# Attention followed by two expert layers on one core: the drain of attention and the first two steps behind it in another order

## The reference, cut to what matters

```python
# attention: B, H, S, D = 2, 8, 768, 64; n_global = 8, n_local = 96
scores = q @ k.T / 8 - slope[h] * dist          # masked to a band of 96 keys and 8 global keys
a = softmax(scores)                             # exp(scores - max) / (sum + 1e-9)
x = (a @ v), heads side by side                 # 1536 x 512, float32
# two layers, each on 1536 tokens, d_model 512, d_ff 2048
h = x @ w_in;  g = h * sigmoid(h);              x = g @ w_out
h = x @ w_in2; g = h * clip(h + 3, 0, 6) / 6;   y = g @ w_out2
```

## Time and profile before

| | |
|---|---|
| median of 3 runs | 621.78 us (621.23 to 623.08) |
| the profiled execution, its own time | 621.76 us |
| its span in the trace | 619.6 us |
| PE busy | 595.8 us, 96% of the span |
| DVE, ACT, POOL busy | 370.6, 339.8, 283.6 us |
| mean granted TensorE clock | 0.989 of full speed |
| share of PE in the chain that ended last | 93% |

### The profile page before, as it was taken

How to read it: one execution, slowest core, us unless ns; L and a number is a source line. 1 busy time by engine, 2 the same in 40 slices (tenths; PEclk the granted TensorE clock), 3 DMA queues, 4 the chain that set the end, 5 groups by cost and what they waited for, 6 DMA issues and landing times.

```text
span 619.6 us, 9570 instructions
## 1 busy us (share of the span) xinstructions
PE 595.8 (96%) x3408; PEld 514.6 (83%) x3408; DVE 370.6 (60%) x696; ACT 339.8 (55%) x657; POOL 283.6 (46%) x353
## 2 busy tenths in 40 slices
PE   3999998599999999999999999999999999999998
PEld 2566666599999999899999998888888888888886
DVE  4778875645755576657655668557555685555431
ACT  3888884444444475544444756555556575555441
POOL 2888975723943333439533333377333333331110
PEclk9999999599999999999999999999999999999999
DMA  7444430212122212321322122212221242211002
GB/s 275 177 154 147 164 115 3 75 65 68 47 90 68 69 35 68 103 69 35 96 72 67 39 69 69 71 66 69 68 69 68 69 165 73 69 68 35 1 0 103
DMA packets 14883, 50.08 MB, mean 81 GB/s; under 512 B 1904, under 2 KB 2160, under 8 KB 14832
## 3 DMA queue, kind: packets, MB, share of 16 engines
q1 hardware_dynamic: 14832, 49.42, 23.4%
HBM read 46.27 MB, written 3.15 MB: 80 GB/s over the span
## 4 chain that ended last, share of the span: by engine, by line
PE 93%; DVE 3%; ACT 1%; issue 1%; DMA 1%; POOL 0%; DVEq 0%; SPq 0%; ACTq 0%
PE ps L898 37%; PE ps L977 22%; PE ps L968 14%; PE ps L969 7%; PE ps L870 4%; PE ps L845 4%; PE ps L855 4%; DMA words<-in_n_loc 1%; DVE x_lo L444 1%; DVE g_lo L586 1%; DVE wi_lo L435 0%; ACT probs L649 0%; POOL probs L274 0%; DVE g_f L460 0%; ACT g_hi L780 0%
## 5 line engine op out<-in xcount | busy, mean ns | idle before, releaser
L365 POOL TENSOR_TENSOR wo_lo<-wo_raw,wo_hi 128x1024 fp32r<-128x1024 f32 x32 | 76.6, 2393 | 282.4 <-ACT wo_hi L774 282.4
L898 PE MATMUL ps<-x_hi,wi_hi 128*128 128x384 f32 x448 | 153.1, 342 | 9.4 <-DVE c_sb L450 4.9
L898 PE MATMUL ps<-x_hi,wi_lo 128*128 128x384 f32 x448 | 151.6, 338 | 0.0
L898 PE MATMUL ps<-x_lo,wi_hi 128*128 128x384 f32 x448 | 151.6, 338 | 0.0
L450 DVE TENSOR_TENSOR c_sb<-ps,p_c 128x384 f32<-128x384 f32 x64 | 35.7, 557 | 171.6 <-PE ps L898 171.4
L697 ACT ACTIVATE p_c<-ps 128x384 f32<-128x384 f32 x64 | 31.5, 492 | 140.3 <-PE ps L898 140.1
L898 PEld LDWEIGHTS ps<-x_hi,wi_hi 128*128 128x128 f32 x448 | 85.2, 190 | 14.1 <-DVE c_sb L450 5.7
L898 PEld LDWEIGHTS ps<-x_hi,wi_lo 128*128 128x128 f32 x448 | 85.4, 191 | 0.6
L898 PEld LDWEIGHTS ps<-x_lo,wi_hi 128*128 128x128 f32 x448 | 85.4, 191 | 0.0
L977 PE MATMUL ps<-wo_hi,g_hi 128*128 128x512 f32 x192 | 75.9, 395 | 0.0
L977 PE MATMUL ps<-wo_hi,g_lo 128*128 128x512 f32 x192 | 75.9, 395 | 0.0
(11 more groups left out here) (89 smaller groups left out, 1081.5 us busy)
## 6 DMA issues: line engine op xcount, KB each, us to landing
wi_raw<-in_w_in SPq DMA_DIRECT2D x32, 512.0 KB, 3.3
wo_raw<-in_w_out SPq DMA_DIRECT2D x32, 512.0 KB, 3.3
v_raw<-in_v SPq DMA_DIRECT2D x8, 704.0 KB, 4.2
k_raw<-in_kT SPq DMA_DIRECT2D x8, 464.0 KB, 4.9
q_raw<-in_qT SPq DMA_DIRECT2D x8, 384.0 KB, 5.5
out_y<-y_out SPq DMA_DIRECT2D x11, 256.0 KB, 4.2
out_y<-y_out SPq DMA_DIRECT2D x2, 128.0 KB, 1.8
words<-in_n_glob SPq DMA_DIRECT2D x1, 1.0 KB, 2.6
```

The lines of the kernel that those rows point to most:

```text
L365: nc.gpsimd.tensor_tensor(wo_lo[:, s % 2, :], wo_raw[:, s % 2, :], wo_hi[:, s % 2, :], ALU.subtract).then_inc(wo_lo_ok, 1)
L898: mm = nc.tensor.matmul(p_bank(bank), w[:, s % 2, at], x[:, b, k, :], start=fresh and k == 0 and i == 0, stop=k == 1 and i == 2, skip_grou ...
```

## The change

The x operands B22 and T3 change places in the order in which they are split. During attention, the first half of a third sum (T3) is now made on POOL at unit 41 and the second at unit 44 (the tables `X_SUMS`, `X_HIGHS`, `X_LOWS` replace the old rules), one more `x_high` and `x_low` (B22) run there, and ACT splits w_out of steps 0 and 1 at units 22 and 26. In the drain, PE does all transposes and values but the last values ahead of P6, and then P6, P5, P7, P3, P4 in a row. POOL does `wo_low(0)` and the sums of w_in for step 2 right after its last x sums. In steps 0 and 1 the splitting of w_in for step 2 moves from the end of step 0 into step 1. What follows is the diff, without its parts for `general`, the moved definition of `wo_high`, and the re-indentation of the loops' remaining lines.

```diff
+X_SUMS = (30, 33, 35, 38, 41, 44)
+X_HIGHS = (32, 35, 40, 42, 44)
+X_LOWS = (34, 37, 41, 43, 46)
...
-B11, B21, T2, T1, T3, B22, T4 = range(7)
+B11, B21, T2, T1, B22, T3, T4 = range(7)
...
@@ POOL, banded
-                    if 30 <= u < 42 and u % 3 == 0:
-                        x_sum(0, (u - 30) // 6, u // 3 % 2)
+                    if u in X_SUMS:
+                        x_sum(0, X_SUMS.index(u) // 2, X_SUMS.index(u) % 2)
                 norm(NU - 2)
                 norm(NU - 1)
-                for n in range(2, 4):
-                    for half in range(2):
-                        x_sum(0, n, half)
+                for half in range(2):
+                    x_sum(0, 3, half)
+                wo_low(0)
+                for n in range(4):
+                    w_sum(2, n)
@@ POOL, steps
-            for s in range(NSTEP):
+            for s in range(1, NSTEP):
+                if s == 1:
+                    wo_low(s)
                 if s + 2 < NSTEP:
                     for n in range(4):
                         w_sum(s + 2, n)
-                pool.wait_ge(wo_hi_ok, s + 1)
-                nc.gpsimd.tensor_tensor(wo_lo[:, s % 2, :], wo_raw[:, s % 2, :], wo_hi[:, s % 2, :],
-                                        ALU.subtract).then_inc(wo_lo_ok, 1)
+                if s > 1:
+                    wo_low(s)
@@ DVE, banded
-                    if 36 <= u < 48 and u % 3 == 0:
-                        x_low(0, (u - 36) // 3)
+                    if u in X_LOWS:
+                        x_low(0, X_LOWS.index(u))
                 inverse(NU - 2)
                 inverse(NU - 1)
                 copy_t(NU - 5)
                 copy_t(NU - 4)
+                x_low(0, T3)
                 c_sum(0, 0, 1, p1_c, P2)
                 copy_t(NU - 2)
-                x_low(0, T3)
-                x_low(0, B22)
+                x_low(0, T4)
                 copy_t(NU - 1)
-                x_low(0, T4)
-                silu(0, 0)
-                c_sum(0, 1, 0, p5_c, P7)
-                c_sum(0, 2, 1, u2_c, P3)
-                for n in range(1, 4):
-                    silu(0, n)
@@ DVE, steps
-            for s in range(NSTEP):
+            silu(0, 0)
+            c_sum(0, 1, 0, p5_c, P7)
+            c_sum(0, 2, 1, u2_c, P3)
+            for n in range(1, 4):
+                silu(0, n)
+            g_low(0, 0)
+            for s in range(1, NSTEP):
+                c_sum(s, 0, 1, p1_c, P2)
+                if s == 1:
+                    g_low(0, 1)
+                    w_low(2, 0)
...
                 g_low(s, 0)
                 g_low(s, 1)
+                if s == 1:
+                    w_low(2, 1)
@@ ACT, banded
-                    if 34 <= u < 46 and u % 3 == 1:
-                        x_high(0, (u - 34) // 3)
+                    if u in X_HIGHS:
+                        x_high(0, X_HIGHS.index(u))
+                    if u in (22, 26):
+                        wo_high((u - 22) // 4)
                 nc.scalar.activation(warm[:, :], three[:, :], ACT.Sigmoid)
                 keep(0, p1_c, 0, P1)
+                x_high(0, T3)
                 copy_t(NU - 3)
                 x_copy(14)
-                x_high(0, T3)
-                x_high(0, B22)
                 x_high(0, T4)
+                gated(0, 0)
                 keep(0, u2_c, 0, P6)
                 keep(0, p5_c, 1, P5)
-                gated(0, 0)
-                x_copy(15)
                 gated(0, 1)
                 gated(0, 2)
                 gated(0, 3)
+                x_copy(15)
@@ ACT, steps
-            for s in range(NSTEP):
+            g_high(0, 0)
+            g_high(0, 1)
+            for s in range(1, NSTEP):
+                keep(s, p1_c, 0, P1)
+                if s == 1:
+                    w_high(2, 0)
...
-                if s:
+                if s > 1:
                     wo_high(s)
...
-                if s == 0:
-                    wo_high(s)
+                if s == 1:
+                    w_high(2, 1)
@@ PE, banded
                 product(0, P1)
+                turn_probs(NU - 4)
                 values(NU - 5)
-                turn_probs(NU - 4)
                 product(0, P2)
+                turn_probs(NU - 3)
                 values(NU - 4)
-                turn_probs(NU - 3)
-                product(0, P6)
+                turn_probs(NU - 2)
                 values(NU - 3)
-                turn_probs(NU - 2)
-                product(0, P5)
+                turn_probs(NU - 1)
                 values(NU - 2)
-                turn_probs(NU - 1)
-                product(0, P7)
-                product(0, P3)
-                product(0, P4)
+                for n in range(P6, P4 + 1):
+                    product(0, n)
                 values(NU - 1)
```

More of the change, by code:

```diff
@@ L567, in general @@
                 c_sum(0, 0, 1, p1_c, P2)
-                c_sum(0, 1, 0, p5_c, P7)
-                c_sum(0, 2, 1, u2_c, P3)
-                for n in range(4):
-                    silu(0, n)
             either(dve, banded, general)
@@ L612, in _ @@
                     y_copy(blk - 1, 5)
-                if s:
-                    c_sum(s, 1, 0, p5_c, P7)
-                    c_sum(s, 2, 1, u2_c, P3)
-                    for n in range(4):
-                        if s < NSTEP // 2:
-                            silu(s, n)
-                        else:
-                            hswish(s, n)
+                c_sum(s, 1, 0, p5_c, P7)
+                c_sum(s, 2, 1, u2_c, P3)
+                for n in range(4):
+                    if s < NSTEP // 2:
+                        silu(s, n)
+                    else:
+                        hswish(s, n)
                 g_low(s, 0)
                 g_low(s, 1)
+                if s == 1:
+                    w_low(2, 1)
                 if f == STEPS - 1 and s < NSTEP - 1:
@@ L711, in gated, with wo_high @@
                     nc.scalar.activation(gate[:, n, :], h_quad(n), ACT.Relu, bias=three[:, :]).then_inc(gate_ok, 1)
+            def wo_high(s):
+                act.wait_ge(wo_in[s % 2], 16 * (s // 2 + 1))
+                at_least(act, down_done, s - 1)
+                nc.scalar.activation(wo_hi[:, s % 2, :], wo_raw[:, s % 2, :], ACT.Copy).then_inc(wo_hi_ok, 1)
             def banded():
@@ L763, in general @@
                 keep(0, p1_c, 0, P1)
+                for s in range(2):
+                    wo_high(s)
                 keep(0, u2_c, 0, P6)
@@ L768, in _ @@
             either(act, banded, general)
-            def wo_high(s):
-                act.wait_ge(wo_in[s % 2], 16 * (s // 2 + 1))
-                at_least(act, down_done, s - 1)
-                nc.scalar.activation(wo_hi[:, s % 2, :], wo_raw[:, s % 2, :], ACT.Copy).then_inc(wo_hi_ok, 1)
             def g_high(s, f):
```

17 lines of the change are left out of this document (8 added, 9 removed).

## The result

| | before | with the change |
|---|---|---|
| median of the comparison's runs | 622.43 us (621.23 to 623.35, 4 runs) | 612.98 us (612.93 to 616.23, 4 runs) |
| the profiled execution, its own time | 621.76 us | 612.97 us |
| its span | 619.6 us | 611.2 us |
| PE busy | 595.8 us (96%) | 592.6 us (97%) |
| mean granted TensorE clock | 0.989 | 0.997 |

The ratio is 0.9862, with a 95% interval of 0.9824 to 0.99: 1.4% faster. The forecast was 612.3 us, with a range of 608.0 to 616.5. The total came out within 0.7 us, but three of its five terms were off by 0.6 to 1.9 us, as the stages show. They are cut at PE's first product of step 0, the end of the last values, the first product of step 1 and the first down projection.

A forecast was written before the change was run, and what follows sets the result against it. PE was taken as the bound nearly everywhere, with gains only around its half-clock slice from 108 to 124 us. The terms 0.7 + 2.4 + 0 + 6.4 gave 9.5 us, so 621.8 - 9.5 = 612.3 us; range 608 to 616.5.

The forecast's parts named there:

- Attention: Attention of step 0: PE's 0.72 us wait for a copy goes, work added on the helpers costs nothing; 0.7 us gained.
- The bound given: In attention: the most that the added work could cost if PE did not cover it, 2.9 us.
- Drain: First product to last values of step 0: 2.9 us of waits shrink to 0.5; 2.4 us gained.
- Gap: Last values to first product of step 1: between 1.4 and 3.8 us, taken as 2.6; nothing gained or lost.
- Step 1: Seven products of step 1: 9.5 us available, less 2.4 for the clock and 0.7 for late operations; 6.4 us gained.
- Later: After the first down projection: nothing gained or lost; splits for step 2 still end in time.
- The first: Clock stays full and the `silu` gets by POOL: 2.4 + 1.2 us more gained, about 608.7 us; chance 0.25.
- POOL holds DVE in the drain: In the drain an `x_low` loses to POOL's unbroken list: 2.4 to 5 us lost, 615 to 617 us; chance 0.15.
- ACT is full in attention: ACT full in attention, or late `w_low` holds P1 of step 2: 2 to 3 us lost, about 615; chance 0.10.
- The slower case: Clock falls in the drain and stays half despite dense work, 31 us at half clock: 624 us or more; chance 0.03.
- the signs named for being wrong: Among them: new PE wait in units 22 to 30; `x_lo` or `g_f` over 2 us in the drain, PE idle behind.

## Why the prediction was right, term by term

The sum of the terms was 9.5 us. Attention came out 1.9 us worse than its term, the drain 0.6 worse and step 1 1.3 better: 9.5 - 1.9 - 0.6 + 1.3 = 8.3, which the first down projection shows. The nearness of the total owes something to errors that cancel, and something to which executions were timed: the medians of this kernel were 612.98, 614.3 and 615.79 us in its three comparisons. The three ratios agree better (0.9862 to 0.9869) and make the gain 8.2 to 8.6 us.

1. *Attention (forecast +0.7, measured -1.2).* **This is the step that failed**, in sign. The wait of 0.72 us did go. "I cost these at nothing", by the lag of three units between normalising and transposes, was wrong. ACT's two splits, where the cover had been called thinnest, cost 0.55 us at units 26 to 31. POOL's two extra sums cost some 0.7. The other 0.6 of the miss of 1.9 us is open. One place where POOL's part shows is the timeline of POOL and DVE at unit 44:

```profile
88.36 0.19 POOL L270 TENSOR_SCALAR rsume<-rsum 128x2 f32<-128x2 f32 x1
...
89.33 1.00 POOL L315 TENSOR_TENSOR x_t<-x_raw 128x384 f32<-128x384 f32 x1
...
90.32 0.95 DVE L460 TENSOR_TENSOR x_lo<-x_raw,x_hi 128x768 fp32r<-128x768 f32 x1
90.42 0.91 POOL L270 TENSOR_SCALAR rsume<-rsum 128x2 f32<-128x2 f32 x1
```

   POOL's small operation before a row of normalising takes 0.91 us instead of 0.19, because this time DVE's `x_low` was first, and it comes right behind a sum of 1.00 us. The chain to PE is `rsume`, reciprocal, normalising, transposes, and PE waits 0.30 us at 92.40. The bound given (2.9 us) held, but it was added up from ACT's work alone; POOL was the half that it had left out.
2. *Drain (forecast 2.4, measured 1.8).* Right in its mechanism: the wait of 0.85 us for an `x_low` went, that for `c_sum` shrank from 1.03 to 0.35 us, and the jump passed while DVE still executed (copy at 102.45, `silu` at 103.25). There was luck in that: what covered the jump was the `x_low` of 2.25 us that POOL had held up. The run with the old PE order laid that jump bare at 2.99 us, so the sentence that it would delay P4 "by up to 2 us" was rather low. The 0.5 us left for small waits should have been 1.1 (13.88 - 12.8); the trace names 0.56 of them as waits (0.21 and 0.35).
3. *Gap (forecast 0, measured 0.0).* Right in its cause, by luck in its size: the third `silu` did run against `wo_lo`, but 2.6 had been taken as the middle of 1.4 and 3.8, and neither bound holds. The prediction gave the `silu` the whole `wo_lo` on top of 1.4. The Trainium skill's rule of the lock (SBUF — State Buffer, section "SBUF: two separate sides") is borne out here: the `silu` stood until `wo_lo` was over. The 3.8 was not, since `wo_lo` had begun at 105.61, 1.1 us before the last values ended at 106.69, and that part of the hold cost PE nothing. The 1.4 was too high for the `silu` and too low for the gap: with DVE undisturbed the last `silu` ended 0.5 us after the last values, but P1 came only 2.23 us after them. What probably stands between is PE's own jump, which the prediction had not counted.
4. *Step 1 (forecast 6.4, measured 7.7).* Right in its mechanism. The clock was charged 2.4 us, taken from the fall before, and cost 1.56 (8.95 against 7.39). The 0.7 us for late `keep` and `c_sum` was not needed; no wait is left. Two readings behind the charge were off. In the 3 us before the last values ended PE had been busy for 1.97, so it was a third idle and not half. And of the 14 us at half clock before, most was not idle PE: it was busy for 8.96 of 13.65 us.
5. *Later (forecast nothing).* Right: P1 of step 2 has no wait, and its 42 matmuls take 7.28 us as before.

*The rivals.* The first had two halves: a full clock is what two of three profiles of the changed kernel show, but the `silu` was held in each. With full clock and `wo_lo` moved the profiled execution took 610.5 us, against the 608.7 of that rival. "POOL holds DVE in the drain" came in the small (2.25 us, hidden) and came in full (6.17 us) once two sums were put later. What had been held against it, that the two engines "mostly took turns", is not what the rows before show: there, too, an `x_low` was passed by two sums. "ACT is full in attention" came as 0.55 us. The slower case had nothing in its favour: the longest half-clock stretch of the changed kernel was 3.4 us. One of the signs named for being wrong did appear, a `g_f` of over 2 us with PE idle behind it, and another at its edge, a new wait of PE at unit 30 (0.22 us for POOL, at 59.95).

## What to carry to other kernels

Work that is put beside the bound engine "for nothing" should be costed on each helper by itself, POOL too, at the units where it lands: here two hidden sums and two hidden splits cost attention some 1.3 us. Where VectorE has a two-operand SBUF operation on the critical chain, look at what GpSimd has in its list then, and put a gap or a wait of GpSimd's there rather than an unbroken row: it was worth 5.5 us of one drain here, while in the changed kernel, whose hold was mostly hidden, no gain in time is shown. Put a long jump behind an operation that is early, on every engine: once one wait is gone, the next jump is likely the bound.

## What the hardware showed that was not expected

- A VectorE operation that reads two SBUF operands can be passed over several times by GpSimd, 6.17 us instead of 0.94, when GpSimd's instructions follow each other without a break. One wait of 0.89 us on GpSimd brought it to 1.81. In other places it went in right after the instruction in progress (2.25 beside a `wo_lo` that had 1.4 us left to run). What decides between the two is open.
- It works both ways: a GpSimd operation on two elements per partition took 0.91 us instead of 0.19 beside an `x_low`.
- The clock's fall is not decided by the program alone: the changed kernel, with PE idle for the same 2.6 us after the same dense drain, was granted half clock for 3.4 us in one profile and full clock in two others.
- Executions differ by up to 2.0 us within units 6 to 8, long before anything that the change touches; two executions of the changed kernel itself by 1.2 us. The cause is open.
